# Idle transposes, a new order of the first slots, and attention with the state's matmuls first

## The reference, cut to what matters

```python
# 1. decayed linear attention, batch 4, 8 heads, 768 tokens, head size 48
for t in range(S):
    state = alpha[:, :, t, :, None] * state + np.einsum('bhd,bhe->bhde', k[:, :, t], v[:, :, t])
    y[:, :, t] = np.einsum('bhd,bhde->bhe', q[:, :, t], state)
# 2. x is y as [4, 768, 384]
theta = x @ w_theta
zr, zi = x * np.cos(theta), x * np.sin(theta)
y = np.einsum('ts,bsd->btd', w_tok_r, zr) + np.einsum('ts,bsd->btd', w_tok_i, zi)
u = x + y
x = u + np.maximum(u @ w_ch, 0.0)
# 3. a gated layer: relu(x @ w_in), one half normalized and mixed over the tokens by w_spatial,
#    the product of both halves @ w_out
```

## Time and profile before

| what | value |
|---|---|
| median of three runs | 603.37 us |
| the profiled execution's own time | 605.39 us |
| its span (first to last instruction) | 603.6 us |
| TensorE busy, matmuls | 583.5 us (97%), 4608 records |
| TensorE busy, weight loads | 554.1 us (92%) |
| VectorE busy | 381.5 us (63%) |
| ScalarE busy | 223.4 us (37%) |
| GpSimd busy | 205.2 us (34%) |
| DMA | 49.53 MB, mean 82 GB/s |

### The profile page before, as it was taken

One profiled execution on the slowest core, in us unless ns is written; L12 is line 12 of the kernel. 1 busy time (PEld: TensorE's weight loads), 2 busy tenths in 40 slices (PEclk: granted clock), 3 DMA queues, 4 the chain that ended last, 5 costly groups with the idle time before them and its releaser, 6 DMA issues.

```text
span 603.6 us, 11147 instructions
## 1 busy us (share of the span) xinstructions
PE 583.5 (97%) x4608; PEld 554.1 (92%) x4608; DVE 381.5 (63%) x594; ACT 223.4 (37%) x411; POOL 205.2 (34%) x178
## 2 busy tenths in 40 slices
PE   3899899999999999999999999999999999999998
PEld 3798798999999999999999989999999999989997
DVE  6799898787787887887844257647043713372232
ACT  2656554443444433433443136423231413131210
POOL 4346444442232323322313045537023701361130
PEclk9999999999999999999999999999999999999999
DMA  7862221152131312420233190200120020002002
GB/s 274 283 207 89 66 81 64 57 171 67 63 109 66 105 67 67 156 81 29 79 105 118 39 339 16 79 0 27 52 79 2 1 79 1 1 0 79 1 1 79
DMA packets 20258, 49.53 MB, mean 82 GB/s; under 512 B 1648, under 2 KB 15216, under 8 KB 19696
## 3 DMA queue, kind: packets, MB, share of 16 engines
q1 hardware_dynamic: 20208, 48.81, 23.3%
HBM read 39.37 MB, written 9.44 MB: 81 GB/s over the span
## 4 chain that ended last, share of the span: by engine, by line
PE 85%; DVE 8%; ACT 3%; POOL 2%; issue 1%; DMA 1%; SPq 0%; DVEq 0%
PE psY L461 21%; PE psY L585 6%; PE psC L493 6%; PE psC L420 5%; PE psS L585 4%; PE psF L585 4%; PE psY L562 4%; PE psS L371 3%; PE psY L572 3%; PE psF L399 3%; PE psF L552 3%; PE psY L552 2%; PE psS L562 2%; PE psC L585 2%; PE psS L572 2%; PE psF L572 2%
## 5 line engine op out<-in xcount | busy, mean ns | idle before, releaser
L1076 POOL TENSOR_TENSOR z_lo<-cos_sin,z_hi 128x768 fp32r<-128x768 f32 x23 | 43.6, 1897 | 100.7 <-ACT z_hi L680 100.7
L1143 POOL TENSOR_TENSOR gated_lo<-u_gated,gated_hi 128x384 fp32r<-128x384 f32 x32 | 32.4, 1012 | 123.6 <-ACT gated_hi L790 123.5
L461 PE MATMUL psY<-tok_r_hi,z_hi 128*128 128x384 f32 x129 | 46.6, 361 | 3.3 <-POOL z_lo L1076 2.2
L1063 POOL TENSOR_TENSOR akq<-akq 128x512 f32<-128x512 f32 x23 | 27.4, 1192 | 60.5 <-DVE akq L846 60.5
L790 ACT ACTIVATE gated_hi<-u_gated 128x384 fp32r<-128x384 f32 x32 | 16.8, 525 | 79.2 <-DVE u_gated L1011 79.2
L841 DVE TENSOR_TENSOR akq<-akq,after 128x512 f32<-128x512 f32 x24 | 43.0, 1791 | 1.2 <-DMA akq<-akq 0.4
L461 PE MATMUL psY<-tok_i_lo,z_hi 128*128 128x384 f32 x129 | 43.2, 335 | 0.0
L461 PE MATMUL psY<-tok_i_hi,z_lo 128*128 128x384 f32 x129 | 43.2, 335 | 0.0
L461 PE MATMUL psY<-tok_r_hi,z_lo 128*128 128x384 f32 x129 | 43.2, 335 | 0.0
L461 PE MATMUL psY<-tok_i_hi,z_hi 128*128 128x384 f32 x129 | 43.2, 335 | 0.0
L461 PE MATMUL psY<-tok_r_lo,z_hi 128*128 128x384 f32 x129 | 43.1, 334 | 0.0
(11 more groups left out here) (236 smaller groups left out, 1769.4 us busy)
## 6 DMA issues: line engine op xcount, KB each, us to landing
akq<-akq SPq DMA_DIRECT2D x23, 770.0 KB, 4.5
v<-v_in SPq DMA_DIRECT2D x24, 192.0 KB, 4.6
x_dram<-u_f SPq DMA_DIRECT2D x8, 576.0 KB, 3.7
x_raw<-x_dram SPq DMA_DIRECT2D x4, 1152.0 KB, 5.1
out<-ot SPq DMA_DIRECT2D x24, 192.0 KB, 1.9
raw_tok_r<-w_tok_rT SPq DMA_DIRECT2D x6, 384.0 KB, 7.0
raw_tok_i<-w_tok_iT SPq DMA_DIRECT2D x6, 384.0 KB, 7.8
raw_sp<-w_spT SPq DMA_DIRECT2D x1, 2304.0 KB, 8.9
```

Of the source, the lines that this page charges most:

```text
L461: mm = pe.matmul(psY[:, j, 0:HALF], Z[s][l][:, q, tile(j)], W[m][:, s, half(h)], start=(s == 0 and q == 0 and n == 0), stop=(s == CHUNKS - ...
L1076: pool.tensor_tensor(Z[c][1][:], trigs[g % 2][:], f(Z[c][0][:]), ALU.subtract).then_inc(z_lo, 1)
L1143: pool.tensor_tensor(GA[1][:, j, half(h)], ug[h][:, j], f(GA[0][:, j, half(h)]), ALU.subtract).then_inc(g_lo, 1)
```

## The change

On TensorE `keep_busy(n)` issues n transposes of the identity into a PSUM bank that nothing reads: 10 behind the wait for the constants, 3 behind the turned keys of chunk 0, which now come ahead of the scores, and 10 behind the scores (WARM). `attend` issues the products with the state first, for all heads, and waits for values and mask only then; the products with the scores follow. On ScalarE the theta split stands behind the first copy of the keys, xT high 1 ahead of the sines, keys 2 behind slot 1, and in slots 7 and 8 the token splits stand ahead of `keep_xT`. On VectorE mask 0 moves ahead of the queries of chunk 1, xT low 1 ahead of product 0, the reduction of slot 5 ahead of the keys of chunk 6; the low part of theta's weight and the low parts of token parts 8 and 9 (in slot 7) come over from GpSimd. On GpSimd the low parts of the token weights each come one slot earlier.

```diff
--- before.py
+++ after.py
@@ -50,7 +50,8 @@
 TILE_OF_SLOT = ((-1, 1, 2), (0, 0, 0), (0, 0, 1), (0, 0, 2), (0, 1, 0), (0, 1, 1))
 
 Z_HIGH, Z_LOW = (0, 1), (2,)
-MID_SPLITS = (6, 7)
+WARM = (10, 3, 10)
+MID_SPLITS = (6, 7, 8, 9)
 SPLITS = ((0, 1), (2,), (3,), (4,), (5,), (6, 7), (), (8, 9), (10, 11)) + ((),) * (BATCH * CHUNKS)
 PASSES = ((0, 0), (0, 1), (1, 0))
 TOKEN_HALVES = (slice(0, 64), slice(64, P))
@@ -386,23 +387,25 @@
 
             def attend(g):
                 s, c = g % 2, g % CHUNKS
-                pe.wait_ge(v_arrived[s], 16 * (g // 2 + 1))
-                pe.wait_ge(masked, g + 1)
                 need(pe, xT_lo, g)
                 need(pe, xT_kept, g)
                 if c:
                     pe.wait_ge(state_made, link(g))
+                if c:
+                    for p in range(PAIRS):
+                        pr = slice(2 * HD * p, 2 * HD * (p + 1))
+                        for rows in TOKEN_HALVES:
+                            pe.matmul(psO[rows, pr], Q[akq_of(g)[0]][:, p, rows], S[c % 2][:, p, :],
+                                      start=(p == 0), stop=False, skip_group_check=True)
+                pe.wait_ge(v_arrived[s], 16 * (g // 2 + 1))
+                pe.wait_ge(masked, g + 1)
                 for p in range(PAIRS):
                     for h in range(2):
                         e = slice(HD * (2 * p + h), HD * (2 * p + h + 1))
                         for rows in TOKEN_HALVES:
                             mm = pe.matmul(psO[rows, e], probs[:, h, p, rows], V[s][:, e],
-                                           start=(p == 0 and h == 0), stop=False, skip_group_check=True)
-                    if c:
-                        pr = slice(2 * HD * p, 2 * HD * (p + 1))
-                        for rows in TOKEN_HALVES:
-                            mm = pe.matmul(psO[rows, pr], Q[akq_of(g)[0]][:, p, rows], S[c % 2][:, p, :],
-                                           start=False, stop=(p == PAIRS - 1), skip_group_check=True)
+                                           start=(c == 0 and p == 0 and h == 0),
+                                           stop=(p == PAIRS - 1 and h == 1), skip_group_check=True)
                 mm.then_inc(attended, 1)
 
             def transpose_x(g):
@@ -448,7 +451,7 @@
                 if k < HALVES:
                     last = k * CHUNKS + s // 2 * 2 + 1
                     if last in MID_SPLITS:
-                        pe.wait_ge(tok_lo_mid, len(MID_SPLITS))
+                        pe.wait_ge(tok_lo_mid, MID_SPLITS.index(last) + 1)
                     else:
                         pe.wait_ge(tok_lo, last + 1 if k == 0 else last + 1 - len(MID_SPLITS))
                 if h == 0:
@@ -494,12 +497,23 @@
                                        start=(j == 0 and k == 0), stop=(j == CT - 1 and k == 2))
                 mm.then_inc(ch_made, 1)
 
+            def keep_busy(count):
+
+                for _ in range(count):
+                    pe.transpose(psY[:, 0, 0:P], ident[:], ident[:])
+
             pe.wait_ge(const_made, 4)
+            keep_busy(WARM[0])
             for c in range(CHUNKS):
+                if c == 0:
+                    turn_k(0)
+                    keep_busy(WARM[1])
                 scores(c)
+                if c == 0:
+                    keep_busy(WARM[2])
                 if c:
                     first_mix(FIRST_UNITS[c - 1], range(CT), Z_LOW)
-                turn_k(c)
+                    turn_k(c)
                 if c == 1:
                     pe.wait_ge(theta_lo, 1)
                 if c:
@@ -705,28 +719,33 @@
 
             act.wait_ge(filled, 7)
             act.activation(warm[:], minus_half[:], ACT.Sin)
-            act.wait_ge(theta_in, 16)
-            act.activation(WT[0][:], raw_theta[:], ACT.Copy).then_inc(theta_hi, 1)
             for c in range(CHUNKS):
-                copy_kT(c)
+                if c != 2:
+                    copy_kT(c)
+                if c == 0:
+                    act.wait_ge(theta_in, 16)
+                    act.activation(WT[0][:], raw_theta[:], ACT.Copy).then_inc(theta_hi, 1)
                 if c:
                     whole_turns(c - 1)
                 if c == CHUNKS - 1:
                     for i in SPLITS[c]:
                         tok_high(i)
                 copy_x(c)
-                if c in (0, CHUNKS - 1):
+                if c in (0, 1, CHUNKS - 1):
                     xT_high(c)
                 if c < CHUNKS - 1:
                     for i in SPLITS[c]:
                         tok_high(i)
                 if c:
                     sines(c - 1)
-                if 0 < c < CHUNKS - 1:
+                if 1 < c < CHUNKS - 1:
                     xT_high(c)
-                if c:
+                if c > 1:
                     z_high(c - 1)
                 keep_xT(c)
+                if c == 1:
+                    copy_kT(2)
+                    z_high(0)
 
             for b in range(BATCH - 1):
                 for c in range(CHUNKS):
@@ -744,9 +763,9 @@
                     if g == CHUNKS:
                         act.wait_ge(ch_in, 16)
                         act.activation(WC[0][:], raw_ch[:], ACT.Copy).then_inc(ch_hi, 1)
-                    keep_xT(g)
                     for i in SPLITS[g]:
                         tok_high(i)
+                    keep_xT(g)
 
             whole_turns(ALL - 1)
             sines(ALL - 1)
@@ -818,7 +837,7 @@
 
         @block.vector
         def _(dve):
-            def decay_keys(g):
+            def decays_back(g):
                 s, loads = akq_of(g)
                 if g == 0:
                     dve.wait_ge(alpha_in, 16)
@@ -829,9 +848,6 @@
                     need(dve, state_made, link(g - 1))
                 dve.tensor_tensor_scan(after[:, ::-1], ALPHA[s][:, ::-1], restart[:, ::-1], 1.0,
                                        ALU.mult, ALU.add).then_inc(after_made, 1)
-                scale_keys(g)
-                need(dve, decayed, g)
-                dve.reciprocal(rtotal[:, 0:SCAN:SEG], AFTER[:, :, 0]).then_inc(rtotal_made, 1)
 
             def scale_keys(g):
                 if g == 0:
@@ -840,7 +856,13 @@
                 s = akq_of(g)[0]
                 dve.tensor_tensor(K[s], K[s], AFTER[:, :, 1:SEG], ALU.mult).then_inc(k_scaled, 1)
 
+            def decay_keys(g):
+                decays_back(g)
+                scale_keys(g)
+
             def decay_queries(g):
+                need(dve, decayed, g)
+                dve.reciprocal(rtotal[:, 0:SCAN:SEG], AFTER[:, :, 0]).then_inc(rtotal_made, 1)
                 s = akq_of(g)[0]
                 dve.wait_ge(rtotal_made, g + 1)
                 dve.tensor_tensor_scan(ALPHA[s], ALPHA[s], rtotal[:, 1:], rtotal[:, 0:1],
@@ -914,6 +936,13 @@
                 dve.scalar_tensor_tensor(out=UF[h][:, m], in0=bank[:, 0:HALF], scalar=0.0, in1=UF[h][:, m],
                                          op0=ALU.max, op1=ALU.add).then_inc(x2_made, 1)
 
+            def tok_low(i):
+                m, pair, cols = tok_part(i)
+                hi, lo = (WR, WI)[m]
+                dve.wait_ge(tok_hi, i + 1)
+                dve.tensor_tensor(lo[:, pair, cols], (raw_r, raw_i)[m][:, pair, cols], f(hi[:, pair, cols]),
+                                  ALU.subtract).then_inc(tok_lo_mid, 1)
+
             dve.wait_ge(restart_made, 1)
             decay_keys(0)
             decay_queries(0)
@@ -921,34 +950,40 @@
             dve.tensor_tensor(Q[0], Q[0], ALPHA[0].rearrange("p (q t) -> p q t", q=PAIRS)[:, :, 0:P],
                               ALU.mult).then_inc(q_scaled, 1)
             decay_keys(1)
+            dve.wait_ge(const_made, 4)
+            mask_scores(0)
             decay_queries(1)
-            dve.wait_ge(const_made, 4)
-            for c in range(CHUNKS):
-                if c != 1:
+            update_state(0)
+            dve.wait_ge(theta_hi, 1)
+            dve.tensor_tensor(WT[1][:], raw_theta[:], f(WT[0][:]), ALU.subtract).then_inc(theta_lo, 1)
+            decays_back(2)
+            xT_low(0)
+            mask_scores(1)
+            scale_keys(2)
+            decay_queries(2)
+            for c in range(1, CHUNKS):
+                if c > 1:
                     mask_scores(c)
+                if c == CHUNKS - 1:
+                    decays_back(c + 1)
+                    reduce_angle(c - 1)
+                    scale_keys(c + 1)
+                    decay_queries(c + 1)
+                    xT_low(c)
+                    multiply_z(c - 1)
+                    continue
                 if c > 1:
                     decay_keys(c + 1)
                     decay_queries(c + 1)
-                if c:
-                    reduce_angle(c - 1)
+                reduce_angle(c - 1)
                 update_state(c)
-                if c == 0:
-                    decay_keys(2)
-                if c == CHUNKS - 1:
-                    xT_low(c)
-                if c:
+                if c > 1:
                     multiply_z(c - 1)
```

(38 more changed lines are left out.)

## The result

The changed kernel took 600.22 us (median of five runs, 600.12 to 605.62) where the kernel before took 603.44 us in the same rounds. The ratio is 0.9934 with a 95% interval of 0.9909 to 0.9960: faster by 0.7%, clear of no change, and less than the 1% that the prediction's chances are given for. The prediction said 599.3 us, 596.2 to 603.2. Four of the five times lie between 600.12 and 600.26 us; the fifth, 605.62, has a mean granted clock of 0.989 on record where the others have 0.997 or 1.00. The profiled execution took 600.12 us (span 598.4) where that of before took 605.39 (603.6): 5.3 us less.

What follows compares the result with a forecast made beforehand. TensorE was taken as the bound from 98 us on, with 16.8 us idle before. Terms 2.0 + 2.0 + 1.1 = 5.1 us off 605.39 gave 600.3, and half the 2.0 us offset to the median 599.3 us; range 596.2 to 603.2.

Steps and rivals of the forecast that it cites:

- Part 1: Idle transposes in slot 0 raise TensorE's clock near 14 us, bringing slot 2's mask to 26.4 us: 2.0 us.
- rival (b): First slots: the clock rises before the scores; 6.0 us in all, 597.4 us with the whole offset; chance 0.17.
- Rival (a): First slots: idle transposes don't bring the clock rise forward; 2.6 us in all, about 601.5 us median; chance 0.22.
- Part 2: VectorE's order in slots 0 and 1: mask 0 ahead of queries 1, theta's low part on VectorE, hidden: 0.
- Slots 2 to 4 keep the gain: VectorE sets the pace there; an earlier mask of slot 2 moves these slots as a whole, shortening none.
- rival (c): Slots 1 to 4: GpSimd's split beside the keys costs 1.45 us each, 5.8 us; 606.6 us median; chance 0.06.
- Part 3: Slot 5: with VectorE's reduction ahead of the keys, TensorE's mix starts at 68.7 instead of 70.70: 2.0 us.
- Part 4: Slot 7: TensorE's 1.10 us wait for GpSimd's token splits goes: 1.1 us, bounds 0 and 1.1.
- Part 5: Attention in all slots: putting the state's records ahead of the scores' brings 0, within +-1.2 us.
- (d): Slots 2 to 4: TensorE or a landing token weight holds them, idle transposes' gain lost; 600.8 us median; chance 0.10.

Runs made afterwards that it cites:

- no_idle: The changed kernel without its 23 idle transposes; 601.92 us, ratio 0.9950 to the kernel before.
- changed_again: The changed kernel unaltered, measured again beside three other runs on one chip; 601.07 us, ratio 0.9927 to the kernel before.
- old_slot7: The changed kernel with the splits of token parts 8 to 11 as before; 601.63 us, ratio 0.9956 to the kernel before.
- idle_alone: The kernel before with the idle transposes alone, and chunk 0's keys turned ahead of the scores; 604.61 us, ratio 0.9988.
- idle_theta: The kernel before with the idle transposes and theta's copy behind the first copy of the keys on ScalarE; 604.38 us, ratio 0.9995.
- attend_alone: The kernel before with attention's new order alone (state's products ahead of the scores'); 604.73 us, ratio 0.9993.
- theta_first: The changed kernel with theta's copy again ahead of the first copy of the keys on ScalarE; 600.41 us, ratio 0.9918 to the kernel before.
- old_attend: The changed kernel with attention in the old order (scores and state in turns); 601.57 us, ratio 0.9944 to the kernel before.
- old_slot5: The changed kernel with VectorE's old order in slot 5 (keys and queries ahead of the reduction); 603.07 us, ratio 0.9964 to the kernel before.
- mask2_early: The changed kernel with mask 2 ahead of product 0 and GpSimd's split of token part 2 not held back; 599.07 us, ratio 0.9908.

## Why the prediction was right, and where its terms were not

The profiled gain of 5.27 us met the sum of 5.1 us, but the closeness is luck: four terms were mis-sized, in opposite directions. The mechanisms, a higher clock in the first slots and two waits removed, were right.

- **Part 1, 2.0 us to mask 2, with 2.9 for a rise before the scores.** Measured 2.75: rival (b)'s case, a rise before the scores. Without the transposes (`no_idle`) 1.46 us of it are gone; of the other 1.29 us a part is a rise of the clock that came 2.2 us earlier in that execution, and the order's own part may be as little as 0.36. In `changed_again` and `old_slot7` the clock fell again in slot 1 and the transposes brought mask 2 nothing, a case that the prediction didn't have. `idle_alone` and `idle_theta` show that the transposes need other parts of the change to be worth anything at the end. The rule of the Trainium skill ("TensorE: Matmul & The Clock Gate", Part 4 (PE-mode transpose)) that the prediction cites against Part 1 is not borne out by these float32 transposes: scores right behind nothing but transposes took 1.16 us. Rival (a) is out; by its number the time would have been 601.5.
- **Part 2, VectorE's order in slots 0 and 1, 0.** In `no_idle`, with slot 1 at 1.2 GHz as before, mask 1 is at 17.02 (18.57 in the kernel before, 18.24 in `attend_alone`), and mask 2 keeps little of it, as above. The low part of theta's weight took 1.83 us on VectorE beside GpSimd's scaling of the queries, not 1.35. With the early rise it isn't hidden, as the prediction had said for that case: in the changed kernel VectorE works from mask 0 (9.95 us) to mask 1 (16.70) without a break, and TensorE waits 1.29 us for VectorE's xT low before the angles at 16.93. In `changed_again` the fall in slot 1 came right behind this wait.
- **Slots 2 to 4 keep the gain.** They lost 0.66 us of it, 0.57 of it between masks 2 and 3, where GpSimd held one scan. That is rival (c)'s mechanism, in one slot, on the scan and not on the keys: it was priced for four slots and 5.8 us.
- **Part 3, 2.0 us.** Measured 1.40, all of it VectorE's order. The product started where the sum had it (7.52 us behind mask 5, put at 7.56), was put at 0.96 us and took 1.50 with GpSimd's scaling beside it. The prediction had priced that contention for the keys and not looked for it at the product.
- **Part 4, 1.1 us.** Measured 1.16 (2.26 less 1.10 us from scores to mix), and 1.1 to 1.4 us by `old_slot7`. Right.
- **Part 5, 0 within +-1.2 us.** It pays 0.03 us a slot, about 0.5 us. The row's 0.19 us a group held 0.02 us that goes away, as the bounds allowed; four groups make 0.08 us, of which the scores' records give about 0.06 back.
- **From the profiled time to the median.** Half the 2.0 us offset of the kernel before was carried over; measured, the changed kernel's median equals its profiled time within 0.1 us. Without that step the forecast would have been the profiled frame's 600.3 us, within 0.1 us. The prediction also took the offset unevenly: 1.0 us off for the forecast, 1.3 for rival (a) (602.8 to 601.5), 1.5 for (d) and 2.0 for (b) and (c); and the upper bound, worked out as it says, is 602.8 + 1.2 - 1.0 = 603.0 us and not 603.2. And (b) stands at 597.4 by its own number, while the chances count almost all of it below 597.3. None of this changes the outcome. The profiled execution of the kernel before was of a middle group (24 runs beside `no_idle` lay between 603.25 and 606.58), that of the changed kernel of the lowest; so the gain depends on which executions are compared: 5.27 us between the two profiles, 3.2 us between the medians of the result, 4.3 us between those beside `changed_again` (605.38 and 601.07), 603.06 - 600.12 = 2.9 us between the lowest times.

Sum as measured between the two profiles: 2.75 - 0.66 + 1.40 + 1.16 + 0.5 = 5.2 us. One thing stays open: by parts undone, the lowest times give 1.25 (transposes), 1.65 (slot 5), 1.36 (slot 7) and 0.5 us (attention), together 4.8, more than the 2.9 us between the lowest times of both kernels, but about what lies between the two profiles. Read on each chip against the kernel before they are 3.8 to 4.4 us, still more than 2.9 to 3.1. Whether the lowest executions of the kernel before had an earlier rise of the clock no profile here shows.

## What to carry to other kernels

Filler on one engine may measure nothing alone and pay with a change of order on another (here 0.2 us of lowest time alone, over 1 us with it); test it together with the order before dropping it. A position in one profile depends on when the clock rose and fell in that execution; before a difference between two profiles is given to a change, look where the clock stood in both. When a step is moved, look beside every VectorE operation with two SBUF operands for a GpSimd operation that now overlaps it: here a scan, a product and the keys each paid 0.5 to 1.5 us (1.95 for 1.22, 1.50 for 0.96, 2.14 for 0.69). With times in groups, compare lowest times and positions in the profile, not medians of a few runs.

## What the runs showed of the hardware

TensorE reached 2.4 GHz by transposes alone: in the changed kernel 13 transposes of a 128x128 identity and four of the keys ran from 3.67 us on, and the scores at 7.92 took 1.16 us. So it was in 7 of the 11 profiled executions with these transposes; in the others the rise came within or behind the scores (1.56 us in `theta_first`, 2.08 us in `old_attend`, `old_slot5` and `mask2_early`). In the three without them the scores took 2.08 us.

It fell again in some executions and not in others. The waits ahead of the falls in the first 75 us were 1.83 us (`idle_alone`), 1.79 (`idle_theta`), 1.40 and 0.61 (the changed kernel), 1.29 (`changed_again`), 1.44 (`old_attend`), 2.16 (`attend_alone`), and in `old_slot7` only 0.89, 0.58 and 0.32 us. The same wait of 1.29 us brought no fall in the changed kernel's first profile. A fall on the path cost some 1.5 us in `changed_again` and `old_attend` and 2.2 us of mask 2 in `old_slot7`, where it lasted from 14.4 to 21.3 us.

The granted clock of a stretch is no sign of the rate ahead of the first rise: it reads 1.00 up to 28.4 us in the kernel before, whose matmuls of 384 columns took 0.52 us there. Behind it, it tells the fall: from 18 to 20 us it reads 0.50 in `changed_again`, with the same 0.52 us.
